# Attention of a fused kernel: one step's order on PE, VectorE and ScalarE rewritten, the mix spread over four steps

## What is computed

```python
# attention, window of 128 keys back, slope per head
scores = scale * q @ k.T + bias            # masked outside 0 <= i - j < 128
attn = exp(scores - max); attn = attn / (sum(attn) + 1e-9)
x = attn @ v                               # (B, S, 512)
# token mix of rank 32, then an MLP
u = x + (x.T @ U @ V).T
x = u + relu(u @ w_ch1) @ w_ch2            # 512 -> 2048 -> 512
# gated MLP with a spatial product
h = relu(x @ w_in); u, v = split(h)
v = w_spatial @ norm(v) + b_spatial
out = (u * v) @ w_out
```

## Time and profile before

| | |
|---|---|
| median of three runs | 790.97 us |
| profiled execution, its own time | 789.44 us |
| its span | 787.7 us |
| PE / DVE / ScalarE / GpSimd busy, share of the span | 97% / 38% / 33% / 14% |
| PE busy from 220 us to the end (568 us) | 564.04 us |
| attention, first `values` to first `up` matmul | 16.83 to 169.64 us |
| PE's waits for `xt` (turn back) up to 215 us | 0.7 us, once |

### The profile page before, as it was taken

One profiled execution on the slowest core, in us unless ns is written; L12 is line 12 of the kernel. 1 busy time (PEld: TensorE's weight loads), 2 busy tenths in 40 slices (PEclk: granted clock), 3 DMA queues, 4 the chain that ended last, 5 costly groups with the idle time before them and its releaser, 6 DMA issues.

```text
span 787.7 us, 12405 instructions
## 1 busy us (share of the span) xinstructions
PE 760.7 (97%) x4584; PEld 648.0 (82%) x4584; DVE 297.9 (38%) x823; ACT 258.5 (33%) x654; POOL 110.9 (14%) x95
## 2 busy tenths in 40 slices
PE   6998988889999999999999999999999999999998
PEld 4665666668888999888888888888889899999998
DVE  6877677742111313111131113111447427425432
ACT  5765656542323112110111102122424233342422
POOL 1211112244444000000000000022601010000100
PEclk9999999999999999999999999999999999999999
DMA  5332222202323000000000000011200010000101
GB/s 169 107 92 92 90 75 90 97 28 81 107 83 118 1 1 1 1 1 1 0 0 0 0 0 0 13 44 55 68 16 1 9 53 0 33 27 0 60 1 61
DMA packets 24688, 32.98 MB, mean 42 GB/s; under 512 B 2768, under 2 KB 11984, under 8 KB 24656
## 3 DMA queue, kind: packets, MB, share of 16 engines
q1 hardware_dynamic: 24656, 32.56, 13.2%
HBM read 27.83 MB, written 4.72 MB: 41 GB/s over the span
## 4 chain that ended last, share of the span: by engine, by line
PE 88%; DVE 7%; issue 3%; DMA 0%; DVEq 0%; ACT 0%; POOL 0%; SPq 0%; POOLq 0%
PE bank L1116 8%; PE bank L1118 8%; PE bank L1117 8%; PE bank L1130 6%; PE bank L1132 6%; PE bank L1131 6%; PE wide L1008 4%; DVE pt L719 3%; PE bank L1226 2%; PE bank L1228 2%; PE bank L1227 2%; PE bank L1105 2%; PE bank L1103 2%; PE wide L1132 2%; PE wide L1130 2%
## 5 line engine op out<-in xcount | busy, mean ns | idle before, releaser
L811 DVE SCALAR_TENSOR_TENSOR rl<-bank,rh 128x512 fp32r<-128x512 f32 (+1 forms) x80 | 51.0, 638 | 310.8 <-ACT rh L544 310.8
L544 ACT ACTIVATE rh<-bank 128x512 fp32r<-128x512 f32 (+1 forms) x80 | 44.4, 555 | 310.8 <-PE bank L1118 310.8
L1116 PE MATMUL bank<-uh,w1h 128*128 128x512 f32 (+1 forms) x320 | 117.9, 369 | 0.0
L1117 PE MATMUL bank<-uh,w1l 128*128 128x512 f32 (+1 forms) x320 | 117.7, 368 | 0.0
L1118 PE MATMUL bank<-ul,w1h 128*128 128x512 f32 (+1 forms) x320 | 117.7, 368 | 0.0
L1130 PE MATMUL bank<-rh,w2h 128*128 128x512 f32 (+1 forms) x240 | 88.5, 369 | 0.0
L1131 PE MATMUL bank<-rh,w2l 128*128 128x512 f32 (+1 forms) x240 | 88.3, 368 | 0.0
L1132 PE MATMUL bank<-rl,w2h 128*128 128x512 f32 (+1 forms) x240 | 88.3, 368 | 0.0
L465 ACT ACTIVATE sc<-sc,mn 128x256 f32<-128x256 f32 (+1 forms) x144 | 66.9, 468 | 36.4 <-DVE mn L710 36.4
L1116 PEld LDWEIGHTS bank<-uh,w1h 128*128 128x128 f32 x320 | 60.4, 189 | 10.0
L1118 PEld LDWEIGHTS bank<-ul,w1h 128*128 128x128 f32 x320 | 60.3, 189 | 10.0
(11 more groups left out here) (159 smaller groups left out, 1482.7 us busy)
## 6 DMA issues: line engine op xcount, KB each, us to landing
qkraw<-qk SPq DMA_DIRECT2D x32, 288.0 KB, 3.0
out_t<-tok SPq DMA_DIRECT2D x16, 288.0 KB, 2.1
vraw<-v_n SPq DMA_DIRECT2D x16, 256.0 KB, 2.7
w1raw<-w SPq DMA_DIRECT2D x16, 256.0 KB, 2.9
w2raw<-w SPq DMA_DIRECT2D x16, 256.0 KB, 2.6
w1raw<-w_in SPq DMA_DIRECT2D x8, 256.0 KB, 2.7
w1raw<-w_sp SPq DMA_DIRECT2D x4, 288.0 KB, 2.8
w1raw<-w_out SPq DMA_DIRECT2D x4, 256.0 KB, 2.6
```

Of the source, the lines that this page charges most:

```text
L544: act.activation(rh[:, j % 2, 0:width(c)], r_ps[j % 2][:, 0:width(c)], ACT.Relu).then_inc(r_hi, 1)
L811: dve.scalar_tensor_tensor(out=rl[:, j % 2, 0:width(c)], in0=r_ps[j % 2][:, 0:width(c)], scalar=0.0, in1=rh[:, j % 2, 0:width(c)], op0=ALU ...
L1116: pe.matmul(o, w1h[:, j, k, :], uh[:, k, 0:w], start=(k == 0), stop=False)
L1117: pe.matmul(o, w1l[:, j, k, :], uh[:, k, 0:w], start=False, stop=False)
```

## The change

The steps keep their work. Moved are:

- DVE: the row sums and the reciprocal of pair `p - 1` (`sums`, a function of its own now) stand at the end of step `p`, one step ahead of the scaling. Copy 2 stands ahead of the scaling. The score of tile 4 stands behind copy 3. `lo_t` stands behind the first four scores.
- PE: transposes 2 stand ahead of `turn_back`. One `mix_up` stands in each of four steps, ahead of `values`: k = 0 and 1 of batch b in steps (b + 1, 2) and (b + 1, 3), k = 2 and 3 in (b + 2, 0) and (b + 2, 1). It waits for copy 3 of the pair, whose bank it takes over.
- ScalarE: `hi_t` stands ahead of `keep_xt`.
- PE and DVE: batch 1 is written out as well, the loop runs over batches 2 and 3. `HEADROOM`, the start value of `u_kept`, is 16 instead of 8. The drain has the last two `mix_up` of batch 2.

The diff, cut to its core:

```diff
-HEADROOM = 2 * KD
+HEADROOM = 4 * KD
...
+MIX_STEP = {2: (1, 0), 3: (1, 1), 0: (2, 2), 1: (2, 3)}
...
 # ScalarE, step
+                if i == 2 and not first:
+                    hi_t(b - 1)
                 if two:
                     keep_xt(*back(b, i, 2))
-                if i == 2 and not first:
-                    hi_t(b - 1)
...
 # VectorE, step
                 if one:
                     keep_pt(*back(b, i, 1), 0)
                     keep_pt(*back(b, i, 1), 1)
-                if i == 2 and not first:
+                score(b, i, range(0, AFTER_X))
+                if i == 2 and (whole or b >= 1):
                     lo_t(b - 1)
-                score(b, i, range(0, AFTER_Z))
-                if not first or i >= 2:
+                if one:
+                    keep_pt(*back(b, i, 1), 2)
+                if two:
                     normalise(*back(b, i, 2))
-                if not first or i >= 1:
-                    keep_pt(*back(b, i, 1), 2)
+                if one:
                     keep_pt(*back(b, i, 1), 3)
-                score(b, i, range(AFTER_Z, NT))
-                if not first:
-                    if i >= 2:
-                        add_u(b - 1, 2 * i - 4, pt_ps)
-                        add_u(b - 1, 2 * i - 3, pt_ps)
+                score(b, i, range(AFTER_X, NT))
+                if whole or b >= ago:
+                    add_u(b - ago, k, pt_ps)
+                if one:
+                    sums(*back(b, i, 1))
...
 # PE, turn and step
-                if f < 2 and not (isinstance(b, int) and b == 0):
-                    if i == 2:
-                        pe.wait_ge(u_kept, HEADROOM + (b - 1) * 2 * KD + KD)
-                    elif i == 3:
-                        pe.wait_ge(u_kept, HEADROOM + b * 2 * KD)
+                if f < 2 and mixed is not None:
+                    pe.wait_ge(u_kept, mixed)
...
                 scores_z(b, i)
+                if one:
+                    turn(*back(b, i, 1), 2)
                 if two:
                     turn_back(*back(b, i, 2))
                 if one:
-                    turn(*back(b, i, 1), 2)
                     turn(*back(b, i, 1), 3)
                 scores_y(b, i)
                 if two:
                     turn_x(*back(b, i, 2))
+                if whole or b >= ago:
+                    pe.wait_ge(pt_kept, 4 * p)
+                    mix_up(b - ago, k, pt_ps)
                 if one:
                     values(*back(b, i, 1))
-                if not first:
-                    if i == 1:
-                        mix_down(b - 1)
-                    if i >= 2:
-                        mix_up(b - 1, 2 * i - 4, pt_ps)
-                        mix_up(b - 1, 2 * i - 3, pt_ps)
+                if i == 1 and (whole or b >= 1):
+                    mix_down(b - 1)
...
 # PE, drain
+            turn(B - 1, 3, 2)
             turn_back(B - 1, 2)
-            turn(B - 1, 3, 2)
             turn(B - 1, 3, 3)
             turn_x(B - 1, 2)
+            pe.wait_ge(pt_kept, 4 * B * PAIRS)
+            mix_up(B - 2, 2, pt_ps)
             values(B - 1, 3)
+            mix_up(B - 2, 3, pt_ps)
             up(0, 0)
```

More of the change, by code:

```diff
@@ L720, in keep_pt, with sums @@
                                 pt_ps[f % 2][:, :]).then_inc(pt_kept, 1)
-            def normalise(b, i):
-                p, s = b * PAIRS + i, i % 2
+            def sums(b, i):
+                p = b * PAIRS + i
                 dve.wait_ge(exp_done, (p + 1) * NT)
@@ L729, in normalise @@
                 dve.reciprocal(rinv[:, :], den[:, :]).then_inc(rinv_done, 1)
+            def normalise(b, i):
+                p, s = b * PAIRS + i, i % 2
                 dve.wait_ge(rinv_done, p + 1)
@@ L758, in back, with step @@
                 return (b, i - n) if i >= n else (b - 1, i - n + PAIRS)
-            def step(b, i, first=False):
-                if not first or i >= 1:
+            def step(b, i):
+                whole = not isinstance(b, int)
+                one, two = whole or b * PAIRS + i >= 1, whole or b * PAIRS + i >= 2
+                ago, k = MIX_STEP[i]
+                if one:
                     keep_pt(*back(b, i, 1), 0)
                     keep_pt(*back(b, i, 1), 1)
-                if i == 2 and not first:
+                score(b, i, range(0, AFTER_X))
+                if i == 2 and (whole or b >= 1):
                     lo_t(b - 1)
-                score(b, i, range(0, AFTER_Z))
-                if not first or i >= 2:
+                if one:
+                    keep_pt(*back(b, i, 1), 2)
+                if two:
                     normalise(*back(b, i, 2))
-                if not first or i >= 1:
-                    keep_pt(*back(b, i, 1), 2)
+                if one:
                     keep_pt(*back(b, i, 1), 3)
-                score(b, i, range(AFTER_Z, NT))
-                if not first:
-                    if i >= 2:
-                        add_u(b - 1, 2 * i - 4, pt_ps)
-                        add_u(b - 1, 2 * i - 3, pt_ps)
+                score(b, i, range(AFTER_X, NT))
[3 more added lines that the diff above has]
+                    sums(*back(b, i, 1))
             dve.memset(den[:, :], 1.0).then_inc(acc_free, KD)
@@ L797, in _ @@
             for i in range(1, PAIRS):
-                step(0, i, True)
-            with dve.Fori(1, B) as b:
+                step(0, i)
+            for i in range(PAIRS):
+                step(1, i)
+            with dve.Fori(2, B) as b:
                 for i in range(PAIRS):
@@ L822, in _ @@
             keep_pt(B - 1, 3, 1)
+            keep_pt(B - 1, 3, 2)
             normalise(B - 1, 2)
-            keep_pt(B - 1, 3, 2)
             keep_pt(B - 1, 3, 3)
+            add_u(B - 2, 2, pt_ps)
+            sums(B - 1, 3)
+            add_u(B - 2, 3, pt_ps)
             lo_r(0, 0)
@@ L980, in scores_y, with turn @@
                 last.then_inc(qk_done, 1)
-            def turn(b, i, f):
+            def turn(b, i, f, mixed=None):
                 p = b * PAIRS + i
@@ L1066, in back, with step @@
                 return (b, i - n) if i >= n else (b - 1, i - n + PAIRS)
-            def step(b, i, first=False):
-                one, two = not first or i >= 1, not first or i >= 2
+            def step(b, i):
+                whole = not isinstance(b, int)
+                p = b * PAIRS + i
+                one, two = whole or p >= 1, whole or p >= 2
+                ago, k = MIX_STEP[i]
+                last_ago, last_k = MIX_STEP[(i - 1) % PAIRS]
+                last_ago += i == 0
+                mixed = HEADROOM + (b - last_ago) * 2 * KD + 2 * last_k + 2 if whole or b >= last_ago else None
                 if one:
-                    turn(*back(b, i, 1), 0)
-                    turn(*back(b, i, 1), 1)
+                    turn(*back(b, i, 1), 0, mixed)
+                    turn(*back(b, i, 1), 1, mixed)
                 scores_x(b, i)
                 scores_z(b, i)
+                if one:
+                    turn(*back(b, i, 1), 2)
                 if two:
@@ L1082, in step @@
                     turn_x(*back(b, i, 2))
+                if whole or b >= ago:
+                    pe.wait_ge(pt_kept, 4 * p)
+                    mix_up(b - ago, k, pt_ps)
                 if one:
                     values(*back(b, i, 1))
-                if not first:
-                    if i == 1:
-                        mix_down(b - 1)
-                    if i >= 2:
-                        mix_up(b - 1, 2 * i - 4, pt_ps)
-                        mix_up(b - 1, 2 * i - 3, pt_ps)
+                if i == 1 and (whole or b >= 1):
+                    mix_down(b - 1)
             pe.wait_ge(dist_done, 3)
             for i in range(PAIRS):
-                step(0, i, True)
+                step(0, i)
             pe.wait_ge(mix_ready, 1)
-            with pe.Fori(1, B) as b:
+            for i in range(PAIRS):
+                step(1, i)
+            with pe.Fori(2, B) as b:
                 for i in range(PAIRS):
@@ L1134, in down @@
                     last.then_inc(down_done, 1)
-            turn(B - 1, 3, 0)
-            turn(B - 1, 3, 1)
+            mixed = HEADROOM + (B - 2) * 2 * KD + KD
+            turn(B - 1, 3, 0, mixed)
+            turn(B - 1, 3, 1, mixed)
+            turn(B - 1, 3, 2)
             turn_back(B - 1, 2)
-            turn(B - 1, 3, 2)
             turn(B - 1, 3, 3)
             turn_x(B - 1, 2)
+            pe.wait_ge(pt_kept, 4 * B * PAIRS)
+            mix_up(B - 2, 2, pt_ps)
             values(B - 1, 3)
+            mix_up(B - 2, 3, pt_ps)
             up(0, 0)
@@ L1147, in _ @@
             turn_x(B - 1, 3)
+            pe.wait_ge(u_kept, HEADROOM + (B - 1) * 2 * KD)
             down(0, 0)
```

## The result

The changed kernel takes 777.24 us (median of 4 runs, 777.13 to 778.55), the kernel before 790.99 in the runs beside it. The ratio is 0.9829, 95% interval 0.9812 to 0.9846: 13.5 us less. The forecast was 775.6, range 772.5 to 781.5.

The account below looks back on a forecast made before the run. PE, 97% busy, was taken as the bound, with only its attention gaps winnable; terms summed to 16.8 us less, 15.4 after 1.4 allowance: 774.0 profiled, 775.6 on the median, range 772.5 to 781.5.

Parts of the forecast that it names:

- DVE's chain sets the step: Attention step: DVE's work between PE blocks holds PE; moving the sums a step ahead takes 0.82 us off.
- A tie at `xn`: Turn x: PE comes at 4.82 us into the step, xn is there 0.07 us earlier; the forecast's thinnest place.
- allowance: Taken off the gain because of the tie at xn: 0.1 us for each of 14 steps, 1.4 us.
- rival 1: DVE overlaps do not hold in the new order, xn comes late, 0.5 us a step: 781.2 us; chance 0.12.
- Mix ahead of `values`: One mix piece in each of four steps, additions under values: both old stalls go, step with mix 8.29 us.
- `lo_t`: On DVE behind four scores: xn at 5.47 instead of 4.82, a stall of 0.65 us three times, 1.95 us.
- The wait for the weights in step (3,3): ScalarE's xt copy waits for the first weights, so PE stalls 3.1 us at turn back.
- Rival 2: Later weight transfers or ScalarE's exponentials hold the last step by as much again as 3.1 us: 779 us; chance 0.08.
- The blocks' own lengths: PE's unheld blocks in an attention step sum to 7.67 us without mix, 8.29 us with it.
- The drain: After step (3,3): the step without scores taken at 5.1 us, between its blocks' 3.85 and 3.1 more.
- The bill: From values(0,0) to the first up matmul: 152.8 us becomes 136.0, 16.8 less, or 15.4 after the allowance.
- Copy 2, the third, ahead of the scaling: On DVE: adds 0.60 us ahead of xn but takes it away behind it.

Follow-up runs that it names:

- sums_back: Changed kernel with the row sums and reciprocal right ahead of the scaling again, the rest as changed: 787.26 us, ratio 0.9961.
- sums_only: Kernel before with the row sums and reciprocal one step ahead and nothing else: 780.89 us, ratio 0.9876.
- mix_back: Changed kernel with two mix pieces behind values in steps 2 and 3 again (PE and VectorE): 781.52 us, ratio 0.9891.
- fill_wait: Changed kernel with transposes 2 of step (3,3) made seven times while PE waits for the xt copy: 776.59 us, ratio 0.9830.
- copy2_weights: Changed kernel with copy 2 behind scaling, transposes 2 behind turn back, first weight conversion behind the drain's xt copy: 771.49 us, ratio 0.9768.
- changed_again: The changed kernel unaltered, measured once more beside two other runs: 777.51 us, ratio 0.9826.

## Why the prediction was right, and where it was off

- *DVE's chain sets the step, and the sums are 0.82 us of it*: right. `sums_back` and `sums_only` give 10 and 9.8 us for that part alone. One reading behind it was wrong: "busy only 38% there and elsewhere". 38% is DVE's share of the whole span; in attention it is 28.60 of 40 us, 72%, and 31.88, 80%, with the change. So DVE's amount of work is not far behind there, which the forecast's own count of 7.4 us in a step of 8.3 says too.
- *A tie at `xn`, with 0.1 us a step as allowance*: the tie was won, no wait in any step but those with `lo_t` and the drain's. The allowance of 1.4 us was not needed there; it covered part of an error made elsewhere. The row at 102.20 shows why rival 1 fell: copy 2 is 0.69 us long and the scaling starts 0.60 behind its start. The overlap holds in the new order. The section of the Trainium skill that was weighed ("VectorE: DVE Perf Modes", "The DRAIN you can't avoid") was quoted by half: it adds that a next operation that is not held starts earlier, and that is what these rows show.
- *Mix ahead of `values`, additions under them*: right, no wait for `tok` is left in attention; `mix_back` puts its worth at 7 to 8 us in the steps.
- *`lo_t`*: forecast 0.65 us three times, measured 0.74.
- *The wait for the weights in step (3,3)*: forecast 3.1 us, measured 2.9 (3.8 in another execution). Rival 2 held that it might be as much again; the up phase had no new gap.
- *The blocks' own lengths*: this is the term that was mis-sized. Transposes 0 and 1 were taken from the row at 97.63, 0.87 us; that pair follows a mix down. In the chain they take 1.02 behind `values` (61.62, against 0.87 at 89.76), in the kernel before as well (128.85 to the scores at 129.88 in PE's timeline). By their starts in the timeline most of the difference is one of bookkeeping:

```profile
61.55 1.09 PE L1005 MATMUL bank<-ident,sc 128*128 128x128 f32 x8
62.58 0.93 PE L971 MATMUL bank<-qkraw 64*128 64x128 f32 x8
...
89.59 1.04 PE L1005 MATMUL bank<-ident,sc 128*128 128x128 f32 x8
90.56 0.93 PE L971 MATMUL bank<-qkraw 64*128 64x128 f32 x8
```

  From start to start the pair takes 1.03 us behind `values` and 0.97 behind a mix down. The chain starts a block at the modelled end of the one ahead, and at 89.76 this end lies 0.17 us behind the real start. Taken out of its place, the row at 97.63 loses that piece. The mix piece was taken as the 0.62 us after which DVE starts; from its start to the start of `values` it is 0.72. So steps take 7.82 instead of 7.67 and 8.54 instead of 8.29: eleven steps behind `values` with 0.15 each and ten mix pieces with 0.1, 2.65 us. The three steps with `lo_t` add 0.5 more (the longer wait, and turn x at 0.86 instead of 0.79 behind it).
- *The clock*: the forecast took PE at full clock throughout. The wait that it forecast lowered it, 1.6 us more, as `fill_wait` shows (1.8 against the blocks of another step). That is the missing step: a wait of 3 us was priced at its own length. Step (3,3) took 4.67 us more than one with mix, where 3.1 was forecast.
- *The drain*: forecast 2.05 + 5.1 + 2.05 + 0.62 = 9.8 us from values(3,2) to the up matmul, measured 10.1 (147.45 to 157.58).
- *The bill* up to the first up matmul: forecast 136.0 + 1.4 allowance = 137.4, measured 157.58 - 16.55 = 141.0. The difference of 3.6 is 2.65 for the blocks, 0.5 for the steps with `lo_t`, 1.6 for step (3,3) and 0.3 for the drain, less 1.4 allowance. Attention also begins 0.3 us earlier (16.55 against 16.83): the fifth tile's score no longer stands ahead of the first `values`. 15.4 - 3.6 + 0.3 is 12.1, against 12.3 measured; the 0.2 lie behind the first up matmul. That matmul was forecast at about 154 and came at 157.58.
- *The median, 775.6 against 777.24*: here luck helped. The sum is off by 3.1 us (774.0 against 777.13 for the profiled executions). The forecast added the 1.5 us by which the kernel before's median lies above its profiled execution; in the changed kernel that distance is 0.1 us, and so only 1.6 of the 3.1 show. The later executions of the kernel before tell what the 1.5 may be: with a mean granted clock of 0.999 or 1.0 they took 789.25 to 790.14 us, with 0.995 to 0.998 they took 790.7 to 792.44. The profiled one, at 1.0, is of the first kind; the changed kernel's, at 0.998, already holds its fall.
- *Copy 2, the third, ahead of the scaling*: costed at nothing for the path, and it is nothing there; but I did not say that its old place would be better. It makes `xn` later by 0.6 us, which the three steps with `lo_t` feel: 0.9 us (`copy2_weights`).

## What to carry to other kernels

Where two engines hand work to and fro in one step, write the step as a chain with times from its first row, and move out of it whatever is needed only a step later: small operations of 0.2 us count there by their whole time, although the engine's share of the whole span is 38% (in this stretch it is 72%: look at the stretch, not at the average). When the chain has become shorter than the bound engine's blocks, look at once for what the faster step runs into: here a conversion of weights that nobody needed yet, in the queue of the engine that feeds the next step. And take the length of a block from start to start, behind the neighbour that it will have.

## What the runs showed of the hardware

- In the profiled executions a single wait of 2.9 us (and of 3.8, in `changed_again`) on PE was followed by some 3 us at a granted clock of 0.50; one of 2.0 us, in `sums_only` at 149.21, was not: turn back behind it took 0.77 us, as at full clock. But in the same execution the clock fell in the middle of attention behind waits of 0.40 and 0.66 us, and the same waits one step earlier left it at 1.00. One execution of the changed kernel kept a mean clock of 1.0. A wait's length alone does not tell whether the clock falls.
- The pair of transposes takes 1.03 us from start to start behind `values`, whose matmuls are 128*64 in the timeline, and 0.97 behind the mix down, whose are 128*128. Why was not tried.
- From the end of values(3,1) to the start of the `xt` copy, with the issue of two loads, the first weights' transfer and their conversion between, 5.1 us went by in the changed kernel's profiled execution and 6.1 in that of `changed_again`.
